# Where the output sums of a head are read out of PSUM, and which engine divides them

## The chip, the cores and the metric

One core of one Trainium2 chip. The metric is the device time of one execution in microseconds (us), the median of several runs. Names of engines: PE is TensorE (matrix products), PEld its weight loads, DVE is VectorE, ACT is ScalarE, POOL is GpSimd, SP is SyncE, which issues the loads.

## The reference

Sixteen heads of bucketed attention, then a dense mixture of experts, then a routed one. The change touches the attention alone:

```python
scores = scale * np.matmul(q, k.transpose(0, 1, 3, 2))
scores = np.where(mask, scores, -1000000000.0)      # mask: same hash bucket
scores = scores - np.max(scores, axis=-1, keepdims=True)
attn = np.exp(scores)
attn = attn / (np.sum(attn, axis=-1, keepdims=True) + 1e-09)
return np.matmul(attn, v).astype(np.float32)
```

q, k and v are 2 x 8 heads of 768 rows of 64. The result, turned so that a token's eight heads stand side by side, is the input x (1536 x 512) of the experts.

## The kernel before

The program is written by hand for each engine: an engine runs its instructions in the order of the code, and semaphores, counted up by `then_inc` and awaited by `wait_ge`, tie the engines together.

**The attention** takes the first 270 us. Head g (0 to 15) is done in six steps, one for each tile of 128 query rows; i counts steps over all heads (96), q is the tile in its head. `head_pairs` runs heads two at a time: the first and the last pair are written out, the six pairs between are one hardware loop over j. In step i the engines do this, each in its own order:

- PE: `scores` of tile i+2 (768 keys, into one of two PSUM areas psS, once `exp` of tile i has read it), `turn` (six transposes of tile i's probabilities, in two halves into psT), for some steps the hash products of a coming head (`match_patterns`, `hash_tokens`), then `values` of tile i-1: 18 products of the turned probabilities with V, into psO. psO is a single PSUM bank; it holds, for the six tiles of one head, 64 output columns and one column D with the sum of the probabilities.
- ACT: `exp` of a tile, the high half of the turned probabilities (`take_probsT`, L712, two halves), one-hot codes of a coming head (`one_hot`, L719 and L721), and in two steps of a head the rounding of k and q (L697, L700).
- DVE: `take_probsT_lo` of tile i-1 (L965, two halves), `take_max` of tile i+2 (row_max L971, then row_scale L976 and row_bias L981, which `exp` waits for), in three steps of a head `hash_bits` (L958).
- POOL: for a coming head the low parts of k and q (`split_qk`, L537 to L545), the parts of V (`split_v`, L553 to L559, once the head before the running one has left V's buffer), and after every second head a piece of the first expert's weights (`split_first_w1`, L588 to L592).

**The boundary of a head.** The last `values` of head g-1 runs in step q = 0 of head g. In step q = 1 DVE closes head g-1: `sum_up(g-1, 0)` (L989, denom = (column D + eps) times a scale) stands behind the row maximum, `sum_up(g-1, 1)` (L993, reciprocal of denom) behind row_scale, and `normalise` (L1000, psO times denom into x_attn) behind row_bias. L1000 counts x_ready up. PE may not write psO for head g before that: `values` with q = 0 has

```python
if q == 0:
    pe.wait_ge(v_split, 3 * g + 3)
    reached(pe, x_ready, g)
```

(L1493 to L1495). There are 15 such boundaries inside the attention; head 15 is closed behind the last step, where `turn_x`, which feeds the experts, waits for x_ready = 16 (L1543).

The last pieces of w1 (w1_lo_ready = 7) release the load of w2 and the splitting of x behind the attention.

Of the kernel before, what the change touches and what calls it, by code (L numbers as in the profile page):

```python
# [87 lines left out]
def build(nc, qT, kT, v, proj, consts, gates, w1a, w2a, w1b, w2b, rows, out):  # L88
    ctx = ExitStack()
    with ctx:  # L90
# [3 lines left out]
        def sem(name):  # L94
            return ctx.enter_context(nc.semaphore(name))
# [124 lines left out]
        probsT_lo = [sb(f"probsT_lo{r}", [P, S], fp16, attn) for r in range(2)]  # L220
        denom = sb("denom", [P, QT], fp32, attn)
        qk_in = [sb(f"qk_in{r}", [P, 2, S], fp32, attn) for r in range(2)]
        A = [sb(f"A{r}", [P, 2, S], fp16, attn) for r in range(2)]
# [33 lines left out]
         hash_done, bits_ready, pattern_done, onehot_ready, scores_done, max_ready, scale_ready,  # L257
         bias_ready, probs_ready, turned, probsT_hi_ready, probsT_lo_ready, v_split, pv_done, denom_ready, x_ready) = [sem(n) for n in (
             "consts_in proj_in gates_loaded zeroed setup_ready qk_hi qk_lo q2_ready "
             "hash_done bits_ready pattern_done onehot_ready scores_done max_ready scale_ready "  # L260
             "bias_ready probs_ready turned probsT_hi_ready probsT_lo_ready v_split pv_done denom_ready x_ready").split()]
        v_loaded = [sem(f"v_loaded{r}") for r in range(2)]
# [254 lines left out]
        def _(pool):  # L517
# [30 lines left out]
            def split_v(g, r, turn):  # L548
# [11 lines left out]
                                   ).then_inc(v_split, 1)  # L560

            pool.wait_ge(zeroed, 12)
            pool.wait_ge(blank_ready, 1)
# [33 lines left out]
            for j in range(1, G // 2):  # L597
                split_qk(2 * j, 0)
                split_v(2 * j, 0, j)
                split_qk(2 * j + 1, 1)  # L600
                split_v(2 * j + 1, 1, j)
                split_first_w1(j - 1)
            pool.wait_ge(v_split, 3 * G)

# [344 lines left out]
        def _(dve):  # L949
# [18 lines left out]
            def take_max(i, slot, r, between):  # L968

                dve.wait_ge(scores_done, i + 1)  # L970
                dve.tensor_reduce(row_max[:, slot:slot + 1], psS[r], AX.X, ALU.max  # L971
                                  ).then_inc(max_ready, 1)
                between(0)

                dve.wait_ge(max_ready, i + 1)
                dve.tensor_scalar(row_scale[:, slot:slot + 1], row_max[:, slot:slot + 1],  # L976
                                  -0.5 * Q_MASK * K_MASK, EXP_SCALE, ALU.is_gt, ALU.mult
                                  ).then_inc(scale_ready, 1)
                between(1)
                dve.wait_ge(scale_ready, i + 1)  # L980
                dve.tensor_scalar(row_bias[:, slot:slot + 1], row_max[:, slot:slot + 1],  # L981
                                  row_scale[:, slot:slot + 1], -1.0, ALU.mult, ALU.mult
                                  ).then_inc(bias_ready, 1)

            def sum_up(g, half):

                if half == 0:
                    dve.wait_ge(pv_done, QT * g + QT)
                    dve.tensor_scalar(denom[:, :], psO[:, :, D], EPS, V_SCALE, ALU.add, ALU.mult  # L989
                                      ).then_inc(denom_ready, 1)  # L990
                else:
                    dve.wait_ge(denom_ready, 2 * g + 1)
                    dve.reciprocal(denom[:, :], denom[:, :]).then_inc(denom_ready, 1)  # L993

            def normalise(j, r):
                g = 2 * j + r
                dve.wait_ge(denom_ready, 2 * g + 2)
                dst = x_pairs[:, j, :, r, :] if isinstance(j, int) else \
                    x_pairs[:, bass.ds(j, 1), :, r, :].rearrange("p o q d -> p (o q) d")
                dve.tensor_tensor(dst, psO[:, :, 0:D],  # L1000
                                  denom[:, :].unsqueeze(2).to_broadcast([P, QT, D]), ALU.mult
                                  ).then_inc(x_ready, 1)
# [11 lines left out]
            hash_bits(0, 2)  # L1014
            take_max(0, 0, 0, lambda half: None)
            take_max(1, 1, 1, lambda half: None)
            hash_bits(1, 0)

            def pair(j, first, last):
                for s in range(2 * QT):  # L1020
# [6 lines left out]
                    ends_head = q == 1 and not (first and s == 1)  # L1027
                    between = (lambda half: sum_up(g - 1, half)) if ends_head else lambda half: None
                    if not (last and s >= 2 * QT - 2):
                        take_max(i + 2, (s + 2) % 4, s % 2, between)  # L1030
                    if ends_head:
                        normalise(j - (r == 0), 1 - r)
                    chunk = bucket_chunk(j, s, 1, last)
# [22 lines left out]

            sum_up(G - 1, 0)
            sum_up(G - 1, 1)
            normalise(G // 2 - 1, 1)

# [388 lines left out]
        def _(pe):  # L1449
# [41 lines left out]
            def values(i, g, q, r, head_r):  # L1491
                pe.wait_ge(probsT_lo_ready, 2 * i + 2)
                if q == 0:  # L1493
                    pe.wait_ge(v_split, 3 * g + 3)
                    reached(pe, x_ready, g)  # L1495
                for k in range(QT):
# [427 lines left out]
```

## Time and profile before

| | us |
|---|---|
| median of 3 runs (1391.02 to 1391.27) | 1391.2 |
| time of the profiled execution | 1387.02 |
| its span | 1385.2 |
| PE busy in the span | 1325.8 (96%) |
| DVE busy | 877.3 (63%) |
| ACT busy | 585.7 (42%) |
| POOL busy | 296.9 (21%) |

The profile lists, for each engine, when it was busy and, for each instruction that it did not start at once, how long the engine had sat idle and which instruction released it. A row of a timeline gives start, duration, engine, line, operation, and in brackets such an idle time. Starts of consecutive instructions on one engine can lie closer than their durations, since the next starts while the last one drains; what an instruction costs a busy engine is thus the distance between starts. The shares of the whole span say little on the attention, which is a fifth of it and in which four engines are busy at once.

### The profile page before, as it was taken

What the parts mean: (1) busy time and instruction counts of PE and PEld (TensorE: products, weight loads), DVE (VectorE), ACT (ScalarE), POOL (GpSimd) and SP (SyncE); (2) the same over time, 40 slices, a digit from 0 to 9 for tenths busy, and PEclk for the clock granted to TensorE, in tenths of its full rate; (3) what the DMA queues carried; (4) which work ended last, traced back from release to release, by engine and by line L of the source; (5) the groups of instructions that cost most, each with busy time, mean ns of one, the idle gap of its engine ahead of it and who ended that gap; (6) DMA issues with size and microseconds to landing.
All of it is one profiled execution on the core that took longest, in us unless ns stands there. A gap on an engine that the chain in (4) does not pass through costs nothing.

```text
span 1385.2 us, 25010 instructions
## 1 busy us (share of the span) xinstructions
PE 1325.8 (96%) x9507; PEld 760.7 (55%) x9507; DVE 877.3 (63%) x1555; ACT 585.7 (42%) x909; POOL 296.9 (21%) x210
## 2 busy tenths in 40 slices
PE   6999999798999999999999999999999999999997
PEld 3666666555446545545644554564465455556665
DVE  5999999877557525633743662474275266567984
ACT  6999999753204403411430430232043033225762
POOL 5765666321300300110030030003003000021211
PEclk9999999999999999999999999999999999999999
DMA  8334331114102001101100210110110013268950
GB/s 229 82 88 102 89 80 40 62 42 158 62 24 92 7 1 61 61 0 61 61 0 2 74 45 0 61 61 0 61 61 0 0 62 129 105 215 289 330 203 20
DMA packets 49567, 107.87 MB, mean 78 GB/s; under 512 B 4600, under 2 KB 6776, under 8 KB 49504
## 3 DMA queue, kind: packets, MB, share of 16 engines
q1 hardware_dynamic: 47264, 103.63, 23.2%
q0 software_dynamic: 2240, 3.35, 0.7%
q8 instruction: 45, 0.74, 0.2%
q14 instruction: 18, 0.15, 0.0%
HBM read 93.63 MB, written 17.34 MB: 80 GB/s over the span
## 4 chain that ended last, share of the span: by engine, by line
PE 81%; DVE 10%; issue 4%; ACT 2%; POOL 2%; DMA 1%; SPq 0%; ACTq 0%; DVEq 0%; POOLq 0%
PE ps L1566 14%; PE ps L1569 14%; PE ps L1570 14%; PE ps L1592 10%; PE ps L1594 10%; PE ps L1595 10%; PE ps L1488 2%; DVE probsT_lo L965 2%; DVE row_max L971 2%; ACT probsT_hi L712 1%; PE ps L1498 1%; PE ps L1476 1%; PE ps L1478 1%; DVE x_lo L1043 1%; PE ps L1456 1%
## 5 line engine op out<-in xcount | busy, mean ns | idle before, releaser
L1592 PE MATMUL ps<-x_hi,w_hi 128*128 128x384 f16 x896 | 294.2, 328 | 10.6 <-DVE x_lo L1043 8.9
L1594 PE MATMUL ps<-x_lo,w_hi 128*128 128x384 f16 x896 | 294.3, 328 | 0.0
L1595 PE MATMUL ps<-x_hi,w_lo 128*128 128x384 f16 x896 | 294.2, 328 | 0.0
L1566 PE MATMUL ps<-w_hi,h 128*128 128x512 f16 x768 | 291.0, 379 | 2.3 <-DVE w_lo L1079 2.3
L1570 PE MATMUL ps<-w_hi,h 128*128 128x512 f16 x768 | 291.0, 379 | 0.0
L1569 PE MATMUL ps<-w_lo,h 128*128 128x512 f16 x768 | 291.0, 379 | 0.0
L1199 DVE SCALAR_TENSOR_TENSOR x<-ps,gate_now,x 128x512 f32<-128x512 f32 x84 | 63.1, 751 | 251.8 <-PE ps L1570 250.6
L800 ACT ACTIVATE x1s<-ps 128x384 f32<-128x384 f32 x64 | 30.4, 475 | 326.2 <-PE ps L1595 326.2
L572 POOL TENSOR_TENSOR wf<-wf 128x1024 f32<-128x1024 f32 x8 | 18.9, 2359 | 636.4 <-PE ps L1595 622.0
L821 ACT ACTIVATE h<-parts 128x1152 f16<-128x1152 f32 x64 | 74.4, 1163 | 137.5 <-DVE parts L1157 137.5
L1592 PEld LDWEIGHTS ps<-x_hi,w_hi 128*128 128x128 f16 x896 | 88.2, 98 | 72.0 <-issue 11.7
L1570 PEld LDWEIGHTS ps<-w_hi,h 128*128 128x128 f16 x768 | 75.1, 98 | 90.7
L1566 PEld LDWEIGHTS ps<-w_hi,h 128*128 128x128 f16 x768 | 75.7, 99 | 89.0 <-DVE w_lo L1079 2.7
L1569 PEld LDWEIGHTS ps<-w_lo,h 128*128 128x128 f16 x768 | 75.1, 98 | 86.2
L1595 PEld LDWEIGHTS ps<-x_hi,w_lo 128*128 128x128 f16 x896 | 88.2, 98 | 59.1 <-issue 1.9
L1594 PEld LDWEIGHTS ps<-x_lo,w_hi 128*128 128x128 f16 x896 | 88.1, 98 | 58.5 <-issue 1.4
L965 DVE TENSOR_TENSOR probsT_lo<-ps,probsT_hi 128x384 f16<-128x384 f32 x192 | 97.1, 546 | 2.3 <-ACT probsT_hi L712 1.8
L705 ACT ACTIVATE probs<-ps,row_bias,row_scale 128x768 f32<-128x768 f32 x96 | 96.7, 1008 | 3.9 <-DVE row_bias L981 2.7
L971 DVE TENSOR_REDUCE row_max<-ps 128x1 f32<-128x768 f32 x96 | 91.3, 951 | 8.7 <-PE ps L1478 8.7
L1239 DVE SCALAR_TENSOR_TENSOR h<-parts,h 128x1152 f16<-128x1152 f32 x64 | 87.5, 1368 | 9.3 <-ACT h L821 9.2
L712 ACT ACTIVATE probsT_hi<-ps 128x384 f16<-128x384 f32 x192 | 85.0, 498 | 18.9 <-PE ps L1488 18.7
L1488 PE MATMUL ps<-const,probs 128*128 128x128 f32 x576 | 87.4, 282 | 4.5 <-DVE probsT_lo L965 2.6
(219 smaller groups left out, 2333.3 us busy)
## 6 DMA issues: line engine op xcount, KB each, us to landing
wf<-w1a SPq DMA_DIRECT2D x32, 512.0 KB, 5.8
w_stage_in<-w2a SPq DMA_DIRECT2D x8, 2048.0 KB, 8.8
w_in<-w1b SPq DMA_DIRECT2D x4, 2048.0 KB, 8.6
w_in<-w2b SPq DMA_DIRECT2D x4, 2048.0 KB
w_in_b<-w1b SPq DMA_DIRECT2D x4, 2048.0 KB, 9.9
w_in_b<-w2b SPq DMA_DIRECT2D x4, 2048.0 KB
rows<-blank SPq DMA_DIRECT2D x1, 6682.0 KB, 21.2
qk_in<-qT SPq DMA_DIRECT2D x32, 192.0 KB, 4.0
```

The lines of the kernel that those rows point to most:

```text
L705: act.activation(probs[r][:, :], psS[r], ACT.Exp, bias=row_bias[:, slot:slot + 1], scale=row_scale[:, slot:slot + 1]).then_inc(probs_ready, 1)
L712: act.activation(probsT_hi[r][:, half * HALF:(half + 1) * HALF], psT[half], ACT.Copy).then_inc(probsT_hi_ready, 1)
L965: dve.tensor_tensor(probsT_lo[r][:, keys], psT[half], probsT_hi[r][:, keys], ALU.subtract).then_inc(probsT_lo_ready, 1)
L971: dve.tensor_reduce(row_max[:, slot:slot + 1], psS[r], AX.X, ALU.max).then_inc(max_ready, 1)
L1239: dve.scalar_tensor_tensor(out=h[:, b, 1, i, 1:4, :], in0=now[:, :, :], scalar=0.0, in1=h[:, b, 0, i, 1:4, :], op0=ALU.max, op1=ALU.subtra ...
L1488: last = pe.transpose(psT[half][:, k * P:(k + 1) * P], probs[r][:, keys], ident)
L1566: first = pe.matmul(acc, a_hi, b_hi, start=(m == 0), stop=False)
L1569: pe.matmul(acc, a_hi, b_lo, start=False, stop=False)
L1570: last = pe.matmul(acc, a_lo, b_hi, start=False, stop=(m == n - 1))
L1592: pe.matmul(group_bank(g, role), w_hi, x_hi, start=(opens and kt == 0), stop=False, skip_group_check=not opens)
L1594: pe.matmul(group_bank(g, role), w_hi, x_lo, start=False, stop=False, skip_group_check=not opens)
L1595: last = pe.matmul(group_bank(g, role), w_lo, x_hi, start=False, stop=(kt == 1), skip_group_check=not opens)
```

## The change

The closing of a head is cut in two. DVE, in step q = 1 and now ahead of the row maximum, computes denom and copies the 384 output columns of psO into a new SBUF tile o_sum; the copy counts o_taken up, and it is o_taken that PE's first `values` of the next head awaits. The reciprocal stands between row maximum and row_scale. POOL multiplies o_sum with denom into x_attn, behind its `split_v`; it counts x_ready up, which DVE awaits before it writes denom and o_sum for the next head. The last head is closed as before, by DVE straight from psO.

```diff
+            def normalise(g):
+                pool.wait_ge(o_taken, g + 1)
+                pool.wait_ge(denom_ready, 2 * g + 2)
+                pool.tensor_tensor(x_pairs[:, g // 2, :, g % 2, :], o_sum[:, :, :],
+                                   denom[:, :].unsqueeze(2).to_broadcast([P, QT, D]), ALU.mult).then_inc(x_ready, 1)
...
                 split_qk(2 * j, 0)
                 split_v(2 * j, 0, j)
+                normalise(2 * j - 2)
                 split_qk(2 * j + 1, 1)
                 split_v(2 * j + 1, 1, j)
+                normalise(2 * j - 1)
                 split_first_w1(j - 1)
+            normalise(G - 2)
...
                 dve.tensor_reduce(row_max[:, slot:slot + 1], psS[r], AX.X, ALU.max
                                   ).then_inc(max_ready, 1)
-                between(0)
+                between()
...
-                between(1)
                 dve.wait_ge(scale_ready, i + 1)
...
+            def take_o(g):
+                dve.wait_ge(pv_done, QT * g + QT)
+                reached(dve, x_ready, g)
+                dve.tensor_scalar(denom[:, :], psO[:, :, D], EPS, V_SCALE, ALU.add, ALU.mult
+                                  ).then_inc(denom_ready, 1)
+                dve.tensor_copy(o_sum[:, :, :], psO[:, :, 0:D]).then_inc(o_taken, 1)
+            def invert_sum(g):
+                dve.wait_ge(denom_ready, 2 * g + 1)
+                dve.reciprocal(denom[:, :], denom[:, :]).then_inc(denom_ready, 1)
...
-                    between = (lambda half: sum_up(g - 1, half)) if ends_head else lambda half: None
+                    between = (lambda: invert_sum(g - 1)) if ends_head else lambda: None
+                    if ends_head:
+                        take_o(g - 1)
                     if not (last and s >= 2 * QT - 2):
                         take_max(i + 2, (s + 2) % 4, s % 2, between)
-                    if ends_head:
-                        normalise(j - (r == 0), 1 - r)
...
-                    reached(pe, x_ready, g)
+                    reached(pe, o_taken, g)
```

DVE before, step q = 1 of a head in the loop, from the second half of probsT_lo to the head's closing (ps is PSUM: psT in the first row, psS in the second, psO after; the line numbers are those of the kernel before):

```order
L965 TENSOR_TENSOR probsT_lo<-ps,probsT_hi 128x384 [waits probsT_hi_ready]
L970 REGISTER_ALU
L971 TENSOR_REDUCE row_max<-ps 128x1 [waits scores_done]
L988 ISA
L989 TENSOR_SCALAR denom<-ps 128x6 [waits pv_done]
L976 TENSOR_SCALAR row_scale<-row_max 128x1 [waits max_ready]
L992 ISA
L993 RECIPROCAL denom<-denom 128x6 [waits denom_ready]
L981 TENSOR_SCALAR row_bias<-row_max,row_scale 128x1 [waits scale_ready]
L997 REGISTER_ALU
L1000 ISA [waits denom_ready]
L1000 TENSOR_TENSOR x_attn<-ps,denom 128x6x64
```

DVE after, the same place (line numbers of the changed kernel):

```order
L976 TENSOR_TENSOR probsT_lo<-ps,probsT_hi 128x384 [waits probsT_hi_ready]
L997 ISA
L999 TENSOR_SCALAR denom<-ps 128x6 [waits x_ready,pv_done]
L1001 COPY o_sum<-ps 128x384
L981 REGISTER_ALU
L982 TENSOR_REDUCE row_max<-ps 128x1 [waits scores_done]
L1005 ISA
L1006 RECIPROCAL denom<-denom 128x6 [waits denom_ready]
L987 TENSOR_SCALAR row_scale<-row_max 128x1 [waits max_ready]
L991 TENSOR_SCALAR row_bias<-row_max,row_scale 128x1 [waits scale_ready]
```

denom and the read of the output columns moved ahead of the row maximum, and nothing stands behind row_bias any more.

POOL before, from the splitting of V for one head to that of k and q for the next:

```order
L553 TENSOR_TENSOR V_hi<-V_in,v_scale 128x6x64 [waits q2_ready,pv_done,v_loaded0]
L556 TENSOR_TENSOR V_in<-V_in,v_scale 128x384 [waits v_split]
L559 TENSOR_TENSOR V_lo<-V_in,V_hi 128x6x64 [waits v_split]
L537 TENSOR_TENSOR K<-qk_in,A 64x768 [waits v_split,qk_hi]
L541 TENSOR_TENSOR A<-qk_in,A 64x768 [waits qk_hi,qk_lo]
```

POOL after:

```order
L554 TENSOR_TENSOR V_hi<-V_in,v_scale 128x6x64 [waits q2_ready,pv_done,v_loaded0]
L557 TENSOR_TENSOR V_in<-V_in,v_scale 128x384 [waits v_split]
L560 TENSOR_TENSOR V_lo<-V_in,V_hi 128x6x64 [waits v_split]
L567 TENSOR_TENSOR x_attn<-o_sum,denom 128x6x64 [waits denom_ready,o_taken]
L538 TENSOR_TENSOR K<-qk_in,A 64x768 [waits v_split,qk_hi]
L542 TENSOR_TENSOR A<-qk_in,A 64x768 [waits qk_hi,qk_lo]
```

The division joined POOL's list between V and the next head's k. On PE no instruction moved; only the semaphore in the wait of the first `values` of a head is another.

## Rows read from the trace of the kernel before

**Rows 1.** The table by stretches: busy us (instructions) per engine, 90 to 120 us.

```profile
90.00:120.00 30.00, 27.97 (x339) 18.93 (x337) 28.52 (x69) 27.45 (x50) 19.07 (x15) 1.00 0.32 78
```

**Rows 2.** Groups of instructions, 30 to 290 us: busy, mean ns | idle before, releaser.

```profile
L971 DVE TENSOR_REDUCE row_max<-ps 128x1 f32<-128x768 f32 x90 | 85.6, 951 | 4.8 <-PE ps L1478 4.8
L1498 PE MATMUL ps<-V_hi,probsT_hi 128*128 128x65 f16 x558 | 61.4, 195 | 13.5 <-POOL V_lo L559 7.1 <-DVE x_attn L1000 6.4
```

**Rows 3.** Timeline of DVE around one boundary in the loop.

```profile
97.55 0.94 DVE L971 TENSOR_REDUCE row_max<-ps 128x1 f32<-128x768 f32 x1
...
98.71 0.21 DVE L981 TENSOR_SCALAR row_bias<-row_max,row_scale 128x1 f32<-128x1 f32 x1
...
99.22 1.00 DVE L965 TENSOR_TENSOR probsT_lo<-ps,probsT_hi 128x384 f16<-128x384 f32 x2
100.16 0.96 DVE L971 TENSOR_REDUCE row_max<-ps 128x1 f32<-128x768 f32 x1
101.03 0.15 DVE L989 TENSOR_SCALAR denom<-ps 128x6 f32<-128x6 f32 x1
101.15 0.15 DVE L976 TENSOR_SCALAR row_scale<-row_max 128x1 f32<-128x1 f32 x1
...
101.60 0.56 DVE L1000 TENSOR_TENSOR x_attn<-ps,denom 128x384 f32 x1
102.07 0.41 DVE L958 TENSOR_SCALAR bits<-ps 64x256 bf16<-64x256 f32 x1
102.40 1.00 DVE L965 TENSOR_TENSOR probsT_lo<-ps,probsT_hi 128x384 f16<-128x384 f32 x2
103.70 0.96 DVE L971 TENSOR_REDUCE row_max<-ps 128x1 f32<-128x768 f32 x1 [0.30 <-PE ps L1478]
...
105.02 1.01 DVE L965 TENSOR_TENSOR probsT_lo<-ps,probsT_hi 128x384 f16<-128x384 f32 x2
106.00 0.96 DVE L971 TENSOR_REDUCE row_max<-ps 128x1 f32<-128x768 f32 x1
```

**Rows 4.** Timeline of PE around the same boundary.

```profile
101.03 0.38 PE L1456 MATMUL ps<-qk_stack,proj 128*64 128x256 f32 x1
102.30 0.19 PE L1498 MATMUL ps<-V_hi,probsT_hi 128*128 128x65 f16 x1 [0.89 <-DVE x_attn L1000]
...
103.50 0.71 PE L1488 MATMUL ps<-const,probs 128*128 128x128 f32 x5
```

**Rows 5.** Timeline of ACT around the same boundary.

```profile
102.27 0.99 ACT L705 ACTIVATE probs<-ps,row_bias,row_scale 128x768 f32<-128x768 f32 x1
104.03 0.87 ACT L712 ACTIVATE probsT_hi<-ps 128x384 f16<-128x384 f32 x2 [0.77 <-PE ps L1488]
```

**Rows 6.** Timeline of DVE, the last boundary (head 14).

```profile
256.22 0.95 DVE L971 TENSOR_REDUCE row_max<-ps 128x1 f32<-128x768 f32 x1
...
257.98 1.01 DVE L965 TENSOR_TENSOR probsT_lo<-ps,probsT_hi 128x384 f16<-128x384 f32 x2
259.61 0.96 DVE L971 TENSOR_REDUCE row_max<-ps 128x1 f32<-128x768 f32 x1 [0.62 <-PE ps L1478]
```

**Rows 7.** DVE copies out of PSUM (ns min/median/max), and a POOL product (busy, mean ns | idle).

```profile
L1194 DVE COPY x<-ps x9: 691/692/693, 355.4 to 397.8; 128x512 f32<-128x512 f32 x9
L1103 DVE COPY logit_hi<-ps x1: 251/251/251, 343.1 to 343.1; 128x96 f32<-128x96 f32 x1
L556 POOL TENSOR_TENSOR V_in<-V_in,v_scale 128x384 f32<-128x384 f32 x14 | 11.6, 827 | 1.1
```

**Rows 8.** Timeline of POOL around the same boundary.

```profile
99.61 0.83 POOL L553 TENSOR_TENSOR V_hi<-V_in,v_scale 128x384 f16<-128x384 f32 x1 [1.22 <-PE ps L1502]
...
101.42 0.89 POOL L559 TENSOR_TENSOR V_lo<-V_in,V_hi 128x384 f16<-128x384 f32 x1
108.35 1.64 POOL L537 TENSOR_TENSOR K<-qk_in,A 64x768 f16<-64x768 f32 x1 [6.04 <-ACT A L697]
```

**Rows 9.** DVE's largest group: ns min/median/max, first and last start in us.

```profile
L965 DVE TENSOR_TENSOR probsT_lo<-ps,probsT_hi x192: 539/547/559, 21.9 to 267.3; 128x384 f16<-128x384 f32 x192
```

More of the change, by code:

```diff
@@ L221, in build @@
         denom = sb("denom", [P, QT], fp32, attn)
+        o_sum = sb("o_sum", [P, QT, D], fp32, attn)
         qk_in = [sb(f"qk_in{r}", [P, 2, S], fp32, attn) for r in range(2)]
@@ L257, in build @@
          hash_done, bits_ready, pattern_done, onehot_ready, scores_done, max_ready, scale_ready,
-         bias_ready, probs_ready, turned, probsT_hi_ready, probsT_lo_ready, v_split, pv_done, denom_ready, x_ready) = [sem(n) for n in (
+         bias_ready, probs_ready, turned, probsT_hi_ready, probsT_lo_ready, v_split, pv_done, o_taken, denom_ready, x_ready) = [sem(n) for n in (
              "consts_in proj_in gates_loaded zeroed setup_ready qk_hi qk_lo q2_ready "
              "hash_done bits_ready pattern_done onehot_ready scores_done max_ready scale_ready "
-             "bias_ready probs_ready turned probsT_hi_ready probsT_lo_ready v_split pv_done denom_ready x_ready").split()]
+             "bias_ready probs_ready turned probsT_hi_ready probsT_lo_ready v_split pv_done o_taken denom_ready x_ready").split()]
         v_loaded = [sem(f"v_loaded{r}") for r in range(2)]
@@ L983, in take_max, with normalise_last @@
                                   ).then_inc(bias_ready, 1)
[L985 to L996, printed above, removed]
+            def take_o(g):
[7 more added lines that the diff above has]
+                dve.reciprocal(denom[:, :], denom[:, :]).then_inc(denom_ready, 1)
+            def normalise_last():
+                g = G - 1
+                dve.wait_ge(pv_done, QT * G)
+                dve.wait_ge(x_ready, g)
+                dve.tensor_scalar(denom[:, :], psO[:, :, D], EPS, V_SCALE, ALU.add, ALU.mult).then_inc(denom_ready, 1)
+                invert_sum(g)
                 dve.wait_ge(denom_ready, 2 * g + 2)
-                dst = x_pairs[:, j, :, r, :] if isinstance(j, int) else \
-                    x_pairs[:, bass.ds(j, 1), :, r, :].rearrange("p o q d -> p (o q) d")
-                dve.tensor_tensor(dst, psO[:, :, 0:D],
+                dve.tensor_tensor(x_pairs[:, G // 2 - 1, :, 1, :], psO[:, :, 0:D],
                                   denom[:, :].unsqueeze(2).to_broadcast([P, QT, D]), ALU.mult
@@ L1014, in _ @@
             hash_bits(0, 2)
-            take_max(0, 0, 0, lambda half: None)
-            take_max(1, 1, 1, lambda half: None)
+            take_max(0, 0, 0, lambda: None)
+            take_max(1, 1, 1, lambda: None)
             hash_bits(1, 0)
@@ L1055, in sum_x @@
                                   ).then_inc(sums_dve, 1)
-            sum_up(G - 1, 0)
-            sum_up(G - 1, 1)
-            normalise(G // 2 - 1, 1)
+            normalise_last()
             sum_x(0)
```

## The prediction

> **What bounds the kernel now.** Only the attention is touched, so I began with the table by stretches, to see which engines are full there. In 30 us of it DVE is busy 28.52, PE 27.97, ACT 27.45 and POOL 19.07 [rows 1]: three engines within 4% of each other, so shares can't say which one sets the pace. The second view is the table of groups with the idle time in front of them, which says where PE and DVE stand still. PE has one large wait: 13.5 us before the first product of `values` [rows 2], which is 0.9 us at each of 15 boundaries between heads. DVE has one too, 4.8 us before the row maximum, always for PE's scores [rows 2]. Third, the timelines around one boundary, read side by side. DVE finishes the row maximum, then denom, reciprocal and, at 101.60, the division out of psO; it lasts 0.56, and PE starts `values` at 102.30, 0.14 behind its end, after 0.89 of idling [rows 3, 4]. PE is then late with the scores of the next tile, and DVE, ready at about 103.40, gets them at 103.70: idle 0.30 [rows 3]. So the two waits are one event seen twice. PE loses 0.9 at a boundary, and DVE, which is what the steps are paced by (its instructions follow each other without a gap between boundaries), loses 0.3. The time that can be won is DVE's loss and not PE's: over the attention 14 times 0.30 and once 0.62 [rows 6], together the 4.8 of [rows 2].
>
> **The change, part by part.** I follow the boundary of [rows 3] from 100.16, when DVE has the turned probabilities behind it.
>
> *The copy itself.* No row shows a copy of 384 columns out of PSUM. Two show 96 columns in 251 ns and 512 in 692 [rows 7]: (692 - 251) / 416 = 1.06 ns for a column, so 384 take 692 - 128 x 1.06 = 556 ns. The division that it replaces reads as many columns in 0.56 us [rows 3]. The two are equal, and like the division (101.60 to 102.07) the copy should hold the engine 0.47 us from start to start. A bound from below is 0.25 (the 96 columns), from above 0.69 (the 512). I take 0.47, from the two rows' slope and from the division alike. The Trainium skill ("VectorE: DVE Perf Modes", The TRN2 errata) gives 120 + FD cycles at 0.96 GHz for PSUM to SBUF. An estimate from it is 525 ns for 384 columns; by that the boundary would be some 0.03 us shorter, half a microsecond over the kernel.
>
> *DVE's boundary.* Now: denom 0.12 (start to start, 101.03 to 101.15), the copy 0.47, then the row maximum and what follows. From a row maximum to the next probsT_lo, with hash bits in between, an ordinary step takes 99.22 - 97.55 = 1.67; the reciprocal fits into the gap that this step has between maximum and row_scale, where denom fits now. Sum 0.12 + 0.47 + 1.67 = 2.26. Before it was 102.40 - 100.16 = 2.24 [rows 3]. So the order costs DVE 0.02: the two small instructions no longer both fill the gaps between maximum, scale and bias, but a register instruction and a wait ahead of the division go.
>
> *What is late next.* PE: its last hash product ends at 101.03 + 0.38 = 101.41 [rows 4]. o_taken comes at 100.16 + 0.12 + 0.56 = 100.84, and with the 0.14 from the signal to the product PE could start at 100.98. The hash products cover that, so the 0.89 is gone and `values` starts at 101.41. From there to the turning of the next tile PE needs 103.50 - 102.30 = 1.20, which gives 102.61. But the turning also needs the first half of probsT_lo gone from its bank: DVE starts that at 100.16 + 2.26 = 102.42 and it takes 0.55 [rows 9], so the turning starts at 103.02, and not at 103.50. The scores are done before it, and DVE's next row maximum follows the two halves of probsT_lo without a wait, at 102.42 + 0.94 = 103.36 and not at 103.70. The 0.30 is gone. In the next step DVE now needs 106.00 - 105.02 = 0.98 from probsT_lo to maximum where elsewhere it needs 100.16 - 99.22 = 0.94 [rows 3]: again a little late PE, which also goes. ACT: the high half is taken at 104.03 after an idle 0.77 behind PE's turning [rows 5]; it moves with the turning by 0.48. That is more than DVE gains, so ACT, whose next steps are the fullest of a head, doesn't hold DVE back.
>
> *The later bias.* row_bias now starts at 100.16 + 0.59 + (98.71 - 97.55) = 101.91 and ends at 102.12; before it ended at about 101.55. `exp` awaits it, but ACT was busy with one-hot codes and started only at 102.27 [rows 5]. 0.15 of cover remains. If it were gone there would still be the 0.77 that ACT idles behind that `exp`. I cost this at nothing.
>
> *Sum.* In the loop a boundary gains 0.30 + 0.04 - 0.02 = 0.32, twelve times 3.8 us. In the written-out pairs there is no register instruction to lose: at the last boundary the old way took 257.98 - 256.22 = 1.76 [rows 6], the new one 0.12 + 0.47 + (105.02 - 103.70) = 1.91, so 0.15 more against an idle of 0.62: gain 0.47. The other two, with 0.30 + 0.04 and the same 0.15: 0.19 each, 0.4 together. All 15: 4.7 us. The last head is closed as before, and what follows moves up as a whole.
>
> *POOL.* 15 divisions. A product of this size takes it 0.83 us [rows 7]; it would stand at 102.3, behind V_lo [rows 8], when o_sum (100.84) and the reciprocal (about 101.8) are there. DVE asks for x_ready one head, some 15.7 us, later. Behind it POOL waits 6.04 for ACT in one head of two [rows 8]; in the other the w1 piece and k follow, but POOL idles 1.22 before the next V and is busy 19 of 30 us [rows 1], with 0.83 per head about 20.7. The k, q and V parts are for a head ahead. I cost POOL at nothing; without that slack it would be 15 x 0.83 = 12 us. SP's queue: its loads wait for hash products and splits, which come no later.
>
> *A rule against the change.* DVE's largest group has its 192 instances between 539 and 559 ns [rows 9], while POOL works two thirds of the time beside it: no slowing by POOL is seen, and I take none. The Trainium skill ("GPSIMD Engine Reference", Key points) says that GpSimd shares its SBUF interfaces with VectorE and contends with instructions that have two SBUF inputs or a two-port mode. By that rule the probsT_lo beside the moved division, with one input in PSUM, would be untouched, and the sum is the same by rule and by row; with two SBUF inputs each overlap could have cost up to POOL's own time, the 12 us above.
>
> **The rivals.**
> *PE's whole wait comes back.* The chain of waits passes through `values` at the boundary, and 13.5 us stand before it [rows 2]. If PE paced the steps, the time would be 1391.2 - 13.5 = 1377.7. Against: at every boundary DVE idles only 0.3 afterwards, so an earlier PE meets a full DVE. Something in between (up to 8 us) is possible if the earlier ACT also shortens the ACT-full steps.
> *A smaller gain.* Each 0.1 us that a boundary costs more on DVE (the copy at its upper bound 0.69 instead of 0.47, a semaphore wait that the gaps don't hide, the second semaphore before denom) takes 1.5 us. With 0.15 more: 1391.2 - 4.7 + 2.3 = 1388.8. For: three of the pieces were never run in this order. Here belongs also that the change doesn't free PE everywhere: the table gives V_lo 7.1 of the 13.5 [rows 2], and if V_lo were the true releaser at eight boundaries, half of the gain stayed away, 1388.9. Against: at 102.30 PE starts while V_lo runs until 102.31 [rows 4, 8], the code has V_lo there a head ahead, and the wait is 0.9 in either case.
> *Slower: DVE waits for the sums.* denom and copy now stand in front of the row maximum, 0.87 us earlier than denom did (101.03 - 100.16). They wait for the last `values` of the head, with the row maximum, the bias and thereby `exp` queued behind them. The last `values` is done by 99.61, when it releases POOL [rows 8], so there are 0.55 us to spare. Should it come w us after DVE, each boundary costs w: from w = 4.7 / 15 = 0.31 the gain is gone, with w = 0.6 the kernel ends at 1391.2 - 4.7 + 9.0 = 1395.5. It would need PE 1.15 us later there than now, and the change makes PE earlier.
>
> **How the numbers follow.** The forecast, a gain of 4.7: 1386.5 us against the median of 1391.2; for a profiled execution, 1387.02 - 4.7 = 1382.3, with a span of 1380.5. Its own range, 1385 to 1388.4, has a chance of 0.60. The smaller gain, to nothing at all, has 0.25; the larger one 0.08; the slower case 0.07. A measurement of this kernel tells about 0.2%, 2.8 us, from no change. Above it are the forecast, the larger gain and a little of the smaller one: 0.72. Same: 0.21. Slower: 0.07. The range that should hold 8 times in 10 goes from 1383.5 (the larger gain up to 7.7) to 1391.0 (nearly nothing gained).
>
> **What would show it.** Right: PE's idle before the first product of `values` falls from 13.5 us to under 2; DVE's before the row maximum from 4.8 to under 1; the copy takes 0.55 to 0.57; a head takes 15.4 us instead of 15.7; the late w1 piece and POOL's products show no new wait, and DVE none at denom for POOL. Wrong: DVE idle before denom; `exp` waiting for row_bias in the loop; a copy of 0.7; the head's length unchanged with PE's idle gone, which would mean that ACT or DVE fills in elsewhere.

## The result

| | us | interval or range |
|---|---|---|
| kernel before, median of the comparison | 1391.11 | 6 executions, 1388.82 to 1391.75 |
| changed kernel, median | 1381.24 | 6 executions, 1379.86 to 1383.54 |
| ratio | 0.9935 | 0.9922 to 0.9949 |
| profiled execution, time (span) before | 1387.02 (1385.2) | granted clock over the span 0.993 |
| profiled execution, time (span) after | 1383.54 (1381.7) | granted clock 0.990 |

The median fell by 9.9 us where 4.7 was forecast: a small change (0.7%), but the interval of the ratio is clear of 1. 1381.24 lies below the range of 1383.5 to 1391.0. The two profiled executions differ by only 3.5 us. So there are three numbers, 3.5, 4.7 and 9.9, and the first question is which of them is the change. I took the attention by itself: its end is the start of the last head's division on DVE (L1000 before, L1015 after). The next fence has that row before and after; its columns are min/median/max ns, then the first and last start, and the last start is the end of the attention.

```profile
L1000 DVE TENSOR_TENSOR x_attn<-ps,denom x3: 547/547/558, 242.9 to 270.0; 128x384 f32<-128x384 f32 x3
```
```profile
L1015 DVE TENSOR_TENSOR x_attn<-ps,denom x1: 558/558/558, 264.7 to 264.7; 128x384 f32<-128x384 f32 x1
```

The attention is 5.3 us shorter (269.97 to 264.72). Behind it the same code runs in both kernels. The table by stretches, 270 to 350 us, shows what differs there: columns are the busy us of PE, PEld, DVE, ACT and POOL, then the granted clock, and then the DMA share. Before, after, and one more execution of the changed kernel (run a_third, below):

```profile
270.00:350.00 80.00, 66.93 (x484) 39.70 (x482) 62.20 (x83) 38.34 (x58) 20.90 (x11) 0.91 0.25 87
```
```profile
270.00:350.00 80.00, 72.04 (x487) 41.04 (x488) 59.09 (x81) 36.37 (x56) 17.86 (x10) 0.87 0.29 100
```
```profile
270.00:350.00 80.00, 70.91 (x499) 41.09 (x498) 59.03 (x81) 35.86 (x55) 17.34 (x10) 0.93 0.30 104
```

The profiled execution of the changed kernel had 0.87 of full clock there and was slower behind the attention than before by 1.8 us (1117.0 against 1115.2); a_third, the same code, had 0.93 and a span of 1379.4.

**The predicted rows.** Groups of the changed kernel, 30 to 290 us (busy, mean ns | idle before, releaser), to be read against [rows 2]:

```profile
L1501 PE MATMUL ps<-const,probs 128*128 128x128 f32 x552 | 86.4, 285 | 7.4 <-DVE probsT_lo L976 5.6
L982 DVE TENSOR_REDUCE row_max<-ps 128x1 f32<-128x768 f32 x90 | 85.2, 947 | 0.7
...
L1511 PE MATMUL ps<-V_hi,probsT_hi 128*128 128x65 f16 x558 | 61.7, 196 | 0.1
```

PE's 13.5 us before `values` are 0.1 and DVE's 4.8 before the row maximum are 0.7. PE's idle before its turning grew, that for DVE's probsT_lo from 2.3 to 5.6; the turning in the kernel before was

```profile
L1488 PE MATMUL ps<-const,probs 128*128 128x128 f32 x552 | 84.0, 283 | 4.1 <-DVE probsT_lo L965 2.3
```

That PE now waits for DVE speaks for DVE as the engine that sets the pace; the experiments below put it to the test. The table by stretches, 90 to 120 us, against [rows 1], has DVE at 29.03 of 30:

```profile
90.00:120.00 30.00, 29.33 (x357) 19.01 (x355) 29.03 (x72) 28.35 (x52) 21.28 (x18) 1.00 0.35 86
```

DVE around the boundary, against [rows 3] (start, duration, engine, line):

```profile
98.38 1.00 DVE L976 TENSOR_TENSOR probsT_lo<-ps,probsT_hi 128x384 f16<-128x384 f32 x2
99.31 0.15 DVE L999 TENSOR_SCALAR denom<-ps 128x6 f32<-128x6 f32 x1
99.38 0.54 DVE L1001 COPY o_sum<-ps 128x384 f32<-128x384 f32 x1
99.85 0.94 DVE L982 TENSOR_REDUCE row_max<-ps 128x1 f32<-128x768 f32 x1
100.71 0.17 DVE L1006 RECIPROCAL denom<-denom 128x6 f32<-128x6 f32 x1
...
101.01 0.21 DVE L991 TENSOR_SCALAR row_bias<-row_max,row_scale 128x1 f32<-128x1 f32 x1
101.18 0.42 DVE L969 TENSOR_SCALAR bits<-ps 64x256 bf16<-64x256 f32 x1
101.52 1.00 DVE L976 TENSOR_TENSOR probsT_lo<-ps,probsT_hi 128x384 f16<-128x384 f32 x2
102.45 0.94 DVE L982 TENSOR_REDUCE row_max<-ps 128x1 f32<-128x768 f32 x1
...
103.74 1.01 DVE L976 TENSOR_TENSOR probsT_lo<-ps,probsT_hi 128x384 f16<-128x384 f32 x2
104.81 0.96 DVE L982 TENSOR_REDUCE row_max<-ps 128x1 f32<-128x768 f32 x1
```

PE, against [rows 4]. There is no wait before the first product at 100.50, and a small one before the turning:

```profile
100.19 0.38 PE L1469 MATMUL ps<-qk_stack,proj 128*64 128x256 f32 x1
100.50 0.20 PE L1511 MATMUL ps<-V_hi,probsT_hi 128*128 128x65 f16 x1
...
102.11 1.01 PE L1501 MATMUL ps<-const,probs 128*128 128x128 f32 x6 [0.23 <-DVE probsT_lo L976]
```

ACT and POOL, against [rows 5] and [rows 8]. `exp` starts 0.20 behind row_bias's end of 101.22, right behind the one-hot code that fills ACT until then; POOL's division stands right behind V_lo.

```profile
101.42 0.99 ACT L716 ACTIVATE probs<-ps,row_bias,row_scale 128x768 f32<-128x768 f32 x1
```
```profile
100.58 0.89 POOL L560 TENSOR_TENSOR V_lo<-V_in,V_hi 128x384 f16<-128x384 f32 x1
101.42 0.83 POOL L567 TENSOR_TENSOR x_attn<-o_sum,denom 128x384 f32<-128x384 f32 x1
```

And the new copy over all heads, against the two copies of [rows 7]:

```profile
L1001 DVE COPY o_sum<-ps x15: 540/540/548, 38.2 to 251.7; 128x384 f32<-128x384 f32 x15
```

### The profile page after: what moved, and what is told of

Same layout as the page of the kernel before. It is cut to its first block, busy times and chain, and to the rows that moved or that the text cites. A ratio compares the mean times of both kernels' runs of the same rounds, so it can differ in the third digit from the quotient of the medians.

```text
span 1381.7 us, 25031 instructions
## 1 busy us (share of the span) xinstructions
PE 1334.3 (97%) x9507; PEld 760.8 (55%) x9507; DVE 875.6 (63%) x1555; ACT 586.1 (42%) x909; POOL 308.0 (22%) x225
## 3 DMA queue, kind: packets, MB, share of 16 engines
HBM read 93.63 MB, written 17.34 MB: 80 GB/s over the span
## 4 chain that ended last, share of the span: by engine, by line
PE 82%; DVE 12%; issue 3%; ACT 1%; DMA 1%; SPq 0%; DVEq 0%; POOL 0%; POOLq 0%; ACTq 0%
PE ps L1579 14%; PE ps L1582 14%; PE ps L1583 14%; PE ps L1605 10%; PE ps L1607 10%; PE ps L1608 10%; DVE row_max L982 4%; DVE probsT_lo L976 3%; PE ps L1501 3%; DVE x_lo L1058 1%; PE ps L1489 1%; PE ps L1491 1%; DVE row_scale L987 1%; PE ps L1469 1%; PE ps L1511 1%
```

## The experiments

Two theories. **D**: DVE paces the attention; the boundary gave back DVE's own idling, the gain is some 5 us, and the rest of the 9.9 is spread between executions. **P**: PE's 13.5 us came back in good part (some 10), and the profiled execution merely hid it. e_divides_w1_late has a single execution, the others are medians of several. "Attention end" is read as above from the profiled execution. The ratio with its interval is the comparison's own estimate and not the quotient of the two medians; the two differ by up to 0.1 per cent.

| run | median us (executions) | ratio, interval | span | clock | attention end |
|---|---|---|---|---|---|
| before, first profile | | | 1385.2 | 0.993 | 269.97 |
| b_again | 1388.83 (12) | 0.9996, 0.9985 to 1.0007 | 1389.1 | 0.989 | 270.36 |
| changed, first profile | 1381.24 (6) | 0.9935, 0.9922 to 0.9949 | 1381.7 | 0.990 | 264.72 |
| a_again | 1383.54 (6) | 0.9949, 0.9933 to 0.9964 | 1383.8 | 0.989 | 264.85 |
| a_third | 1381.98 (5) | 0.9942, 0.9928 to 0.9955 | 1379.4 | 0.993 | 264.18 |
| e_late_copy | 1386.79 (12) | 0.9979, 0.997 to 0.9988 | 1379.9 | 0.995 | 268.46 |
| e_copy_twice | 1388.84 (11) | 0.9996, 0.9985 to 1.0006 | 1385.5 | 0.994 | 271.45 |
| e_hash_twice | 1384.19 (7) | 0.9965, 0.9953 to 0.9977 | 1381.7 | 0.993 | 265.07 |
| e_copy_all | 1389.95 (11) | 1.0000, 0.999 to 1.0009 | 1387.6 | 0.991 | 271.08 |
| e_dve_divides | 1408.51 (4) | 1.013, 1.0112 to 1.0147 | 1409.7 | 0.984 | 293.39 |
| e_divides_w1_late | 1405.44 (1) | one execution; kernel before beside it 1386.2 | 1403.6 | 0.989 | 276.30 |

b_again, a_again, e_late_copy and e_dve_divides ran beside 23 executions of the kernel before, median 1389.07; a_third, e_copy_twice, e_hash_twice and e_copy_all beside 24, median 1388.83.

**b_again, a_again, a_third: the two kernels unchanged, again.** No edit.

> The kernel before, unchanged, timed again so that each execution's span and granted clock can be read. Two theories on the gain of 9.9 us, of which the profiled executions show only 5.25 in the attention (the last division starts at 269.97 before and 264.72 after) and 3.5 in the span. Clock theory: the executions of one kernel differ by how much clock TensorE is granted behind the attention; the untraced ones of this kernel will lie near 1391 with a mean clock of 0.990 or less, the one with 1387.02 had 0.993, and span and clock lie on one line of some 1.3 us for 0.001. Work theory: the mean clock is 0.993 in all of them, and the untraced time is longer for another reason.

> The changed kernel, unchanged, timed again. Clock theory: about 1380 at a clock of 0.994 and about 1383 at 0.990, so that at equal clock the distance to the kernel before is 5 to 6 us and the rest of the 9.9 is a difference in granted clock. Work theory: the distance at equal clock is 9 to 10 us, and something behind the attention runs shorter too.

> The changed kernel once more. In the first comparison it was 9.9 us faster than the kernel before (medians of 6 and 6), in the second 5.5 us (6 and 23), while the attention of both profiled executions is 5.2 to 5.5 us shorter. If the gain is the attention's and the rest is which granted clocks the few executions happened to get, this one gives a ratio near 0.996 (5 to 6.5 us), and span minus end of the attention lies on the line of the other profiles: 1115.2 at clock 0.993, 1117.0 at 0.990, 1118.7 and 1118.95 at 0.989, 1111.4 at 0.995. If the change also shortens what follows, the ratio is again near 0.993 and the profile lies below that line.

The kernel before came out at 1387.5 to 1393.4 over 59 executions, median 1388.9; those at a granted clock of 0.993 lie at 1387.5 to 1389.5, those at 0.990 at 1389.8 to 1393.4. The changed kernel: 1380.5 to 1385.6 over 11 later executions, median 1382.4. The gain between these medians is 6.5 us. A line fitted through all 70, with one slope in the clock for both kernels, gives 1.0 us for 0.001 of clock and 6.8 us between the kernels at equal clock, plus or minus 0.7. The first comparison had put the kernel before at a high sample (1391.11) beside three of six executions of the changed one at 0.994. Against 6.5, its 9.9 is 3 us too large and the forecast's 4.7 is 2 too small. The ratios say somewhat more: 9.0 us in the first comparison, 7.1 in that of a_again and 8.1 in that of a_third, with intervals (7.1 to 10.9, 5.0 to 9.3, 6.2 to 10.0) that have 7.1 to 9.3 in common. So the gain is 6.5 to 8 us, by how the executions are put together.

None of the three expectations came quite true, though the clock theory came nearer each time. The executions of the kernel before lie near 1389 and not near 1391, the slope is 1.0 us and not 1.3, and the distance at equal clock is 6.8 where 5 to 6 was expected. The third ratio, 0.9942, fell between the 0.996 of the one theory and the 0.993 of the other; the profile's span behind the attention, which was the second sign, lies with those of the other kernels, as follows.

The profiled executions say where the clock's part lies. Span less attention end: 1119.0 (a_again, 0.989), 1118.7 (b_again, 0.989), 1117.0 (changed, 0.990), 1116.5 (e_copy_all, 0.991), 1115.2 (before, 0.993), 1115.2 (a_third, 0.993), 1116.6 (e_hash_twice, 0.993), 1114.1 (e_copy_twice, 0.994), 1111.4 (e_late_copy, 0.995). These go with the clock and not with the kernel, to about 1.5 us: at 0.993 both kernels have 1115.2, at 0.989 they have 1118.7 and 1119.0. In the attention the clock is 1.00 in all of these, and the end of it repeats within 0.7 us. That the clock is the cause of the scatter is not shown by a run of its own.

**e_late_copy: GpSimd divides, but PE is released as late as before.**

```diff
-                    if ends_head:
-                        take_o(g - 1)
                     if not (last and s >= 2 * QT - 2):
                         take_max(i + 2, (s + 2) % 4, s % 2, between)
+                    if ends_head:
+                        copy_o(g - 1)
```

denom and reciprocal stand in the gaps of take_max as in the kernel before, and the copy where the division stood.

> Only the move to GpSimd, without the early release: denom and reciprocal stand as in the kernel before, the copy to o_sum takes the place of the division behind row_bias, and GpSimd divides. If the early release is what counts: PE's idle before the first product of a head is 0.9 us again, DVE's before the row maximum 0.3, the attention ends as before within 0.5 us, and the time is that of the kernel before, 1389 to 1391. If taking the division off DVE is worth something by itself: 1383 to 1387.

The attention ended at 268.46, 1.5 to 1.9 us before the kernel before's and 3.6 to 4.3 behind the changed kernel's; the median is 2.3 us below before's. Groups, 30 to 290 us:

```profile
L982 DVE TENSOR_REDUCE row_max<-ps 128x1 f32<-128x768 f32 x90 | 85.6, 951 | 4.8 <-PE ps L1496 4.8
...
L1516 PE MATMUL ps<-V_hi,probsT_hi 128*128 128x65 f16 x558 | 61.4, 195 | 11.7 <-DVE o_sum L1006 11.7
```

Neither value that was expected of the attention came, but one between them. DVE's idle is again exactly the 4.8 of [rows 2]. So the early release is what removes it, and it is worth some 4 us. The rest, 1.5 to 1.9, is there without it, and the timeline has its place:

```profile
101.23 0.19 DVE L992 TENSOR_SCALAR row_bias<-row_max,row_scale 128x1 f32<-128x1 f32 x1
101.34 0.55 DVE L1006 COPY o_sum<-ps 128x384 f32<-128x384 f32 x1
```

From row_bias to the copy 0.11; before, from row_bias (101.36) to the division (101.60) 0.24. The division writes to an address that the loop computes, behind a register instruction and a wait; the copy has neither. 12 x 0.13 = 1.6 us: on a full engine this is not free, though it counts as busy nowhere. The three written-out boundaries say which of the two it is. There the kernel before has the same wait but a fixed address, and from row_bias to the division it takes 0.13, as long as to e_late_copy's copy; in the loop it takes 0.23 to 0.25. So the time goes to the computed address, and not to the wait.

**e_copy_twice: DVE's load up.** A second copy of the same columns, into a spare tile, ahead of the first.

```diff
+                dve.tensor_copy(o_twice[:, :, :], psO[:, :, 0:D])
                 dve.tensor_copy(o_sum[:, :, :], psO[:, :, 0:D]).then_inc(o_taken, 1)
```

> The changed kernel with a second copy of the 384 columns into an unused tile, right before the real one, at each of 15 boundaries: 0.47 us more of DVE each from start to start, and o_taken 0.47 later. If DVE sets the pace of the attention: 7 us more than the changed kernel, about 1388 to 1391, attention end near 272. If PE or ACT sets it: 0 to 2 us more.

The attention ended 6.6 to 7.3 us later than in the changed kernel: 15 x 0.47 = 7.1, all of it on the path. The scatter of the attention's beginning can be left out: from the first head's denom to the last head's division this run took 233.42 us, the three profiles of the changed kernel 226.46 to 226.61. The median rose by 6.5 over the changed kernel's 1382.4, which gives the whole gain back.

**e_hash_twice: PE's load up.** One of the hash products that stand ahead of `values` is done twice, 16 more in all (the profile shows each as two rows).

```diff
+                if c == 2:
+                    pe.matmul(psH[0:64, 0:HC], proj2[:, :], qk_stack[r][:, cols], start=True, stop=True)
```

> The changed kernel with the last hash product of each head issued twice, just ahead of the first product of the next head: 0.27 us more of PE at 14 of the boundaries. If DVE sets the pace and PE has slack there since the change (its turning idles 0.23 for DVE behind it, and DVE takes its next maximum without a wait): 0 to 1 us more in the attention. If PE sets the pace: 3.8 us more.

The attention ended at 265.07, 0.2 to 0.9 later, but that comes from the time before the first boundary: from the first head's denom to the last division it took 226.48 us, as in the changed kernel. PE did become later: its scores end 0.13 us before the row maximum that reads them (102.87), where in the changed kernel it was 0.57 (102.45). The slack took in all of it. These two runs decide between D and P: at the boundary a us more on DVE costs a us, and more on PE ahead of `values` costs nothing. One step further on PE has no slack, as the table of steps below shows; load there was not tested.

**e_dve_divides: the early copy, but DVE divides, out of the copy.**

```diff
-                normalise(2 * j - 2)
...
+            def divide(j, r):
+                g = 2 * j + r
+                dve.wait_ge(denom_ready, 2 * g + 2)
+                dve.wait_ge(o_taken, g + 1)
...
+                dve.tensor_tensor(dst, o_sum[:, :, :],
+                                  denom[:, :].unsqueeze(2).to_broadcast([P, QT, D]), ALU.mult
+                                  ).then_inc(x_ready, 1)
```

> Only the early release, without GpSimd: denom and copy ahead of the row maximum as in the change, but DVE divides from o_sum, behind row_bias. PE's idle should be gone as in the change. If DVE sets the pace of the attention, the division costs its 0.47 us (start to start) at each of 15 boundaries, 7 us: 1387 to 1389, about 2 us under the kernel before or level with it. If PE's 13.5 us had been the prize, this kernel would be as fast as the changed one, 1381.

It took 1408.5: D missed it by 20 us and P by 27. The group of the division, and then DVE and POOL at one boundary:

```profile
L1006 DVE TENSOR_TENSOR x_attn<-o_sum,denom 128x384 f32 x12 | 17.0, 1420 | 2.3 <-issue 1.8
```
```profile
91.40 0.22 DVE L988 TENSOR_SCALAR row_bias<-row_max,row_scale 128x1 f32<-128x1 f32 x1
91.77 2.29 DVE L1006 TENSOR_TENSOR x_attn<-o_sum,denom 128x384 f32 x1
```
```profile
91.74 1.89 POOL L596 TENSOR_TENSOR w_hi<-wf,w_scale 128x1024 f16<-128x1024 f32 x1
93.72 2.09 POOL L598 TENSOR_TENSOR wf<-wf,w_scale 128x1024 f32<-128x1024 f32 x1
```

The division met POOL's splitting of a w1 piece, which had started 0.03 us earlier and lasted until 93.63, and ended 0.43 behind that, as if it had run only when POOL's instruction was over. The other five long ones (2.23 to 2.29) ended 0.41 or 0.42 behind the split that was running. At the other boundary of the pair it started at 110.89, when V_lo was ending (110.05 + 0.89), and took 0.56. The delay goes on. PE idles 2.62 for probsT_lo, its products then take 0.24 to 0.25 in place of 0.19, and DVE waits 1.53 for scores:

```profile
94.90 1.37 PE L1510 MATMUL ps<-const,probs 128*128 128x128 f32 x6 [2.62 <-DVE probsT_lo L973]
...
96.77 0.24 PE L1520 MATMUL ps<-V_hi,probsT_hi 128*128 128x65 f16 x1
```
```profile
99.08 0.96 DVE L979 TENSOR_REDUCE row_max<-ps 128x1 f32<-128x768 f32 x1 [1.53 <-PE ps L1500]
```

Over the 15 boundaries the time from row_bias to what follows the division is 21.3 us longer than without the division, and DVE waits 7.6 us for scores where the changed kernel shows no such wait: together the 29 us by which the attention is longer. In the stretches from 60, 90 and 120 us (30 us each) the granted clock was 0.94, 0.94 and 0.89, against 1.00 in the changed kernel. The Trainium skill ("GPSIMD Engine Reference", Key points) has DVE and GpSimd contend where DVE has two SBUF inputs or works in a two-port mode; the trace agrees, and adds the size.

**e_divides_w1_late: the same, with the w1 pieces split behind the last head.**

```diff
-                split_first_w1(j - 1)
-            normalise(G - 2)
+            for k in range(NP):
+                split_first_w1(k)
```

> The kernel in which DVE divides from the copy (e_dve_divides, 1408.5 us), with GpSimd's splits of the first expert's weights moved behind the attention. Its attention is what counts, since the moved splits now stand in front of the experts and lengthen that part by some 20 us. In e_dve_divides the division had a minimum of 0.55, a median of 0.77 and a maximum of 2.29 us; the long ones stand beside such a split. If GpSimd's work holds up a DVE instruction with two SBUF inputs: the maximum falls under 1 us, PE no longer idles 2.6 us behind it, its clock stays at 1.00 in the attention, and the attention ends some 12 us earlier than in e_dve_divides, near 271. If the long ones have another reason (the address that the loop computes, the wait for its semaphores): they stay.

The twelve divisions of the loop took 559 ns on the mean in place of 1420, and the attention ended at 276.30, 17.1 us earlier than in e_dve_divides, so the w1 splitting was the cause of that part. The granted clock was 1.00 in every stretch from 60 to 264 us. (The total fell little: what follows the attention took 11.0 us longer, with the w1 pieces split only now.) The maximum was expected under 1 us and is 1.89. The last division met a split after all, since the moved ones had begun by then:

```profile
263.22 1.89 DVE L1007 TENSOR_TENSOR x_attn<-o_sum,denom 128x384 f32<-128x384 f32 x1
```
```profile
262.81 1.89 POOL L598 TENSOR_TENSOR wf<-wf,w_scale 128x1024 f32<-128x1024 f32 x1
```

It ended at 265.11, 0.41 behind the split's 264.70. The first division (1.42 us) in the same way ended 0.42 behind POOL's product into Q. This bears the reason out: where the splits are gone the long divisions are gone, and where a long POOL product still runs the division is long. The end of the attention was expected at about 271. The timeline shows what was left out of that:

```profile
103.96 0.21 DVE L989 TENSOR_SCALAR row_bias<-row_max,row_scale 128x1 f32<-128x1 f32 x1
104.37 0.56 DVE L1007 TENSOR_TENSOR x_attn<-o_sum,denom 128x384 f32 x1 [0.19 <-issue]
104.85 0.41 DVE L967 TENSOR_SCALAR bits<-ps 64x256 bf16<-64x256 f32 x1
```

From row_bias to the hash bits 0.89, against 0.17 in the changed kernel, so 0.72 here. Over the twelve boundaries of the loop it is 8.6 us, over the three written-out ones, two of them with a long division, 3.9: enough for the 11.7 us by which the attention is longer than the changed kernel's. In the loop 0.36 to 0.41 pass from row_bias to the start of the division (0.65 once), in the written-out pairs, with the same two waits and a fixed address, 0.13.

**e_copy_all: one copy of all 65 columns, denom computed from it in a gap.** It should have saved the 0.07 of denom ahead of the copy, and released psO sooner.

```diff
-                dve.tensor_scalar(denom[:, :], psO[:, :, D], EPS, V_SCALE, ALU.add, ALU.mult
-                                  ).then_inc(denom_ready, 1)
-                dve.tensor_copy(o_sum[:, :, :], psO[:, :, 0:D]).then_inc(o_taken, 1)
+                dve.tensor_copy(o_sum[:, :, :], psO[:, :, :]).then_inc(o_taken, 1)
...
+                    dve.tensor_scalar(denom[:, :], o_sum[:, :, D], EPS, V_SCALE, ALU.add, ALU.mult
+                                      ).then_inc(denom_ready, 1)
```

> A candidate. The copy takes all 65 columns of psO with it (390 elements a partition instead of 384), denom is computed from the copy in the gap between maximum and row_scale, the reciprocal in the gap between row_scale and row_bias, as in the kernel before. Ahead of the row maximum stands only the copy. If DVE sets the pace: the 0.07 us of denom leave each boundary, the two fillers cost 0.04 instead of nothing, so 0.5 to 1 us less than the changed kernel, hard to tell in the time but visible in the attention's end. If the gaps don't hold both: the same as the changed kernel.

It lost the gain: attention end 271.08, 6.2 to 6.9 us later, median 1389.95. First the form of denom over all heads, then DVE and POOL at one boundary:

```profile
L1005 DVE TENSOR_SCALAR denom<-o_sum x15: 150/780/874, 39.0 to 259.4; 128x6 f32<-128x6 f32 x15
```
```profile
101.62 0.84 DVE L1005 TENSOR_SCALAR denom<-o_sum 128x6 f32<-128x6 f32 x1
102.38 0.14 DVE L987 TENSOR_SCALAR row_scale<-row_max 128x1 f32<-128x1 f32 x1
```
```profile
101.55 0.89 POOL L560 TENSOR_TENSOR V_lo<-V_in,V_hi 128x384 f16<-128x384 f32 x1
```

Six elements a partition take 0.15 out of PSUM and mostly 0.78 out of SBUF, and here they end with V_lo, at 102.46 and 102.44. At the last boundary (259.38), with POOL idle, they took 0.16. The expectation named gaps that are too small as the only danger and did not think of POOL.

## Why the prediction was right and wrong

**What bounds the kernel.** Right. DVE paces the steps, PE's 13.5 us was a wait that mostly hid under it, and its going (to 0.1) moved the attention by what DVE had idled and a little more. e_copy_twice and e_hash_twice show it by load, for the boundary.

**The size of a boundary.** 0.32 forecast. From denom to denom over a pair of heads it was 31.47 us before (101.03 to 132.50) and 30.70 after (99.31 to 130.01), so 0.385 a head. Stepping from one probsT_lo to the next shows which terms were off:

| step of DVE | before | after | gain | forecast |
|---|---|---|---|---|
| the boundary (99.22 to 102.40; 98.38 to 101.52) | 3.18 | 3.14 | 0.04 | -0.02 |
| the step behind (to 105.02; to 103.74) | 2.62 | 2.22 | 0.40 | 0.30 |
| the next (to 107.31; to 106.11) | 2.29 | 2.37 | -0.08 | 0.04 |
| the other three (to 115.11; to 113.88) | 7.80 | 7.77 | 0.03 | 0 |

The gains of the table add to 0.39 a head, the forecasts to 0.32: 0.06 and 0.10 more in the first two rows, 0.12 less in the third, 0.03 more in the last. Three terms were mis-sized. denom holds DVE 0.07 ahead of the copy, and not the 0.12 that had been read from its distance to row_scale. The wait of 0.30 was worth 0.37: the bracket counts from the end of the instruction in front, but without a wait the next one starts 0.07 before that end (102.40 to 103.70 is 1.30, without a wait 0.93). The prediction had the numbers for it, 103.36 against 103.70, and summed the bracket. Against this stands the third row: the next row maximum, 0.94 + 0.04 behind probsT_lo before, was to gain 0.04 and came 1.07 behind it. It waits for PE's scores, though the profile puts no bracket there. The last of them, after and before:

```profile
104.50 0.27 PE L1491 MATMUL ps<-A 128*128 128x256 f16 x1
```
```profile
105.69 0.27 PE L1478 MATMUL ps<-A 128*128 128x256 f16 x1
```

They end at 104.77 and 105.96, and the row maximum starts 0.04 later both times (104.81, 106.00), as it does behind the scores at 103.70, where the bracket names them. In the changed kernel it is 0.04 or 0.05 at 14 of the 15 boundaries. The prediction had followed PE to the turning and stopped there. It let PE be less late in the step behind; but the turning now starts behind DVE's probsT_lo (102.11), PE's work from there to the end of the scores takes 2.66 us, and DVE is back at 104.67. The prediction's start of the turning, 103.02, is also 0.05 more than the 102.42 + 0.55 it was made from; the distance from probsT_lo to turning, 0.60 in it, was 0.59. Twelve boundaries give 4.6, and the other three, forecast at 0.9, some 0.6 to 1.0; together 5.2 to 5.6, by the ends of the attention 5.3 (the first pair of profiles) and 5.6 (the means of two and of three).

**The copy.** 540 ns where 556 was forecast, and 0.47 from start to start, as forecast. The Trainium skill's formula ("VectorE: DVE Perf Modes", The TRN2 errata), by which the estimate was 525, comes as near from the other side.

**What is late next, the later bias, POOL.** Right. `values` was to start right behind the hash products and did (100.19 + 0.38 against 100.50, products overlap); the turning has 0.23 of idling behind probsT_lo, as the prediction's order of events had it, though it did not ask what this does one step later; `exp` is not held up by row_bias in the loop. POOL's division waits once, 7.1 us for head 14, with nobody behind it; DVE never waits for x_ready.

**A rule against the change.** It was right that nothing of the changed kernel is slowed by POOL: probsT_lo, the copy and denom read PSUM and keep their times beside it, and so do the reciprocal (0.17) and row_scale (0.15), which read SBUF. But it was treated as a far case, and its price, at most 15 times POOL's 0.83 us, was too low. e_dve_divides and e_copy_all show how near the case is: the two obvious variants of this change fall to it, and in the first the attention is 29 us longer than in the changed kernel, since the division also meets the splits of 1.89 us.

**How the numbers follow.** Here the prediction failed: the mechanism was right, but the step from the gain to a time was not. It put the uncertainty of the base, 1391.2, at nothing without a reason. 4.7 was subtracted from the median of three executions, 1391.2, and the range was made from the mechanism alone, with nothing for how far such a median moves. But executions of this kernel lie 6 us apart from end to end, and go with the clock that they get behind the attention. The sign was in the table of the times before: the profiled execution had 1387.02 and the median 1391.2, 4.2 us apart, seventeen times the 0.25 over which the three lie. Against the median of the 59 later executions, 1388.9, the forecast would have been 1384.2, and the 1382.4 measured is 1.8 below it. The range ought to have reached 3 us further down for that reason alone. So of the 5.2 us between 9.9 and 4.7 the two comparisons' choice of executions is some 3.4 (9.9 against 6.5), the terms of the boundary are 0.6 to 0.9, and about 1 has no cause shown.

**What stays open.** 5.3 to 5.6 us are seen in the attention, 6.5 to 6.8 in the pooled times, and 7.1 or more by the ratios. The 1 to 2.5 us between have no cause that a run shows. They can be scatter: the 6.8 has an interval of 0.7, the attention's own end another 0.7. An open rival is that an earlier end of the attention changes what clock PE gets behind it. Against it, the 6.8 is a distance at equal clock, and at equal clock the profiles of both kernels have the same time behind the attention (1115.2 at 0.993). But these are two pairs of profiles, and an execution's clock is known to 0.001 only, which is 1 us.

## What to carry to other kernels

When one engine waits for another and that one is nearly full itself, price the change by the paced engine's start-to-start times, with the bracketed idle corrected by the overlap that it loses; the waiting engine's own idle (13.5 us here) is not the prize (5.5). Then follow the waiting engine one step further than the wait that goes: here it was late again in the step behind. When VectorE and GpSimd work side by side, leave the VectorE instruction that reads PSUM where it is: in both variants that read a copy in SBUF instead, VectorE waited for GpSimd and the gain was lost. And before subtracting a few us from a median, compare it with the profiled execution: if they are further apart than the runs of the median, the base itself is uncertain by that much, and the range must hold it.

## What the runs showed of the hardware that was not expected

- A DVE product 128x384 with two float32 inputs in SBUF took 0.56 us beside an idle or ending GpSimd, and up to 2.29 us beside GpSimd products of 128x1024: it ended 0.40 to 0.43 behind the one that held it up, in twelve places of the two runs.
- A DVE add-and-multiply (TENSOR_SCALAR) of 128x6 float32 out of SBUF took 0.16 us with GpSimd idle and 0.84 beside GpSimd's V_lo (0.89), ending with it; out of PSUM 0.15 in either case. The reciprocal, also 128x6 out of SBUF, took 0.17 in the changed kernel at 100.71 while V_lo ran (100.58 to 101.47), and row_scale on one element 0.15: not every form that reads SBUF waits.
- From row_bias to a division that writes to a computed address 0.23 to 0.25 us passed in the kernel before, and 0.13 where the address is fixed, with the same wait. With two waits it was 0.36 to 0.41, and again 0.13 with a fixed address.
- A division of 2.29 us on DVE was followed by 2.62 us of idle on PE, and then by products at 0.24 to 0.25 us in place of 0.19; the granted clock of that stretch was 0.94 in place of 1.00.
- The mean granted clock of the 59 executions of the kernel before ran from 0.988 to 0.993, and 0.001 less went with 1.0 us more of 1389.
